# Attention over channels and an expert layer in Strassen form: extras of step 0 moved, sums of batch two made early, the last pair in eight plain products

## Reference

```python
def _attn_ref(q, k, v, tau):                    # q, k, v: 2 x 6016 x 256
    qn = q / (np.linalg.norm(q, axis=1, keepdims=True) + 1e-06)
    kn = k / (np.linalg.norm(k, axis=1, keepdims=True) + 1e-06)
    s = kn.transpose(0, 2, 1) @ qn / tau        # 256 x 256 for each batch
    s = s - s.max(-1, keepdims=True)
    a = np.exp(s)
    a /= a.sum(-1, keepdims=True) + 1e-09
    return (v @ a).astype(np.float32)
def _moe_ref(x, w_in, w_out):                   # x: 12032 x 256, w_in: 256 x 2048
    h = x @ w_in
    g = h * (1.0 / (1.0 + np.exp(-h)))
    return (g @ w_out).astype(np.float32)
```

## Time and profile before

| | |
|---|---|
| Time, median of 3 runs | 1074.22 us (1074.03 to 1078.78) |
| The profiled execution, its time | 1070.89 us |
| Its span | 1069.1 us |
| TensorE busy | 1034.2 us (97%) |
| VectorE busy | 934.1 us (87%) |
| ScalarE busy | 898.7 us (84%) |
| GpSimd busy | 297.6 us (28%) |
| DMA | 197.06 MB, mean 184 GB/s |

### The profile page before, as it was taken

One profiled execution on the slowest core, in us unless ns is written; L12 is line 12 of the kernel. 1 busy time (PEld: TensorE's weight loads), 2 busy tenths in 40 slices (PEclk: granted clock), 3 DMA queues, 4 the chain that ended last, 5 costly groups with the idle time before them and its releaser, 6 DMA issues.

```text
span 1069.1 us, 15160 instructions
## 1 busy us (share of the span) xinstructions
PE 1034.2 (97%) x4584; PEld 851.6 (80%) x4584; DVE 934.1 (87%) x1307; ACT 898.7 (84%) x1580; POOL 297.6 (28%) x323
## 2 busy tenths in 40 slices
PE   9999998989999999999978999999999999999997
PEld 8987776767888888888867777888888888888886
DVE  6887685689889899899899999899899899899898
ACT  7997676778898998898867788898898898988875
POOL 3695231143120121221273662121121211210100
PEclk9999999999999999999999999999999999999999
DMA  9993421397786885876975885885876876975742
GB/s 358 397 366 89 151 92 66 133 265 176 199 194 152 215 196 135 216 176 148 255 150 143 225 193 124 219 188 132 235 173 152 217 173 147 229 168 130 176 134 88
DMA packets 107921, 197.06 MB, mean 184 GB/s; under 512 B 9424, under 2 KB 42448, under 8 KB 107712
## 3 DMA queue, kind: packets, MB, share of 16 engines
q1 hardware_dynamic: 82720, 150.07, 43.2%
q0 software_dynamic: 24544, 45.17, 25.9%
q10 hardware_dynamic: 576, 0.85, 0.2%
HBM read 145.82 MB, written 50.23 MB: 183 GB/s over the span
## 4 chain that ended last, share of the span: by engine, by line
PE 71%; DVE 6%; ACT 3%; issue 3%; DMA 2%; SPq 1%; DVEq 0%; POOL 0%; ACTq 0%; POOLq 0%
PE ps_h L823 12%; PE ps_h L825 12%; PE ps_h L824 12%; PE ps_o L883 6%; PE ps_o L884 6%; PE ps_o L885 6%; PE ps_h L883 5%; PE ps_h L885 5%; PE ps_h L884 5%; DVE t_raw L1584 1%; DVE g_lo L1572 1%; DMA ring<-s_dram 1%; PE ps_o L870 1%; PE ps_o L872 1%; PE ps_o L874 1%
## 5 line engine op out<-in xcount | busy, mean ns | idle before, releaser
L1572 DVE TENSOR_TENSOR g_lo<-h,g_hi 128x512 fp32r<-128x512 f32 (+1 forms) x296 | 205.4, 696 | 24.5 <-ACT g_hi L1206 23.2
L1206 ACT ACTIVATE g_hi<-h 128x512 fp32r<-128x512 f32 (+1 forms) x296 | 182.5, 620 | 10.2 <-PE ps_h L885 3.8
L648 POOL DMA_DIRECT2D out_t_dram<-fl_sb x70 | 61.6, 879 | 437.0 <-ACT fl_sb L1234 428.8
L823 PE MATMUL ps_h<-b_hi,a_hi_mid 128*128 128x512 f32 (+1 forms) x336 | 132.7, 395 | 6.1 <-ACT h L1183 3.1
L825 PE MATMUL ps_h<-b_hi,a_lo_mid 128*128 128x512 f32 (+1 forms) x336 | 130.9, 390 | 0.0
L824 PE MATMUL ps_h<-b_lo,a_hi_mid 128*128 128x512 f32 (+1 forms) x336 | 130.7, 389 | 0.0
L1558 DVE TENSOR_TENSOR h<-ps_h,w 128x512 f32<-128x512 f32 (+1 forms) x96 | 65.2, 679 | 61.5 <-PE ps_h L825 41.7
L883 PE MATMUL ps_h<-g_hi,ring 128*128 128x512 f32 (+1 forms) x264 | 103.7, 393 | 13.5 <-DVE g_lo L1572 7.2
L1606 DVE TENSOR_TENSOR gx_lo<-t_raw,gx_hi 128x1024 fp32r<-128x1024 f32 (+1 forms) x88 | 107.8, 1225 | 0.6 <-ACT gx_hi L1213 0.6
L1584 DVE TENSOR_TENSOR t_raw<-h 128x1024 f32<-128x1024 f32 (+1 forms) x88 | 107.4, 1221 | 0.0
L883 PE MATMUL ps_o<-gx_hi,ring 128*128 128x512 f32 (+1 forms) x264 | 102.2, 387 | 0.7 <-DVE gx_lo L1616 0.4
(11 more groups left out here) (217 smaller groups left out, 2772.7 us busy)
## 6 DMA issues: line engine op xcount, KB each, us to landing
ring<-s_dram SPq DMA_DIRECT2D x88, 640.0 KB, 5.0
ring<-s_dram SPq DMA_DIRECT2D x88, 256.0 KB, 3.1
out_t_dram<-fl_sb POOLq DMA_DIRECT2D x72, 256.0 KB, 6.2
x_raw<-v_t_dram SPq DMA_DIRECT2D x58, 256.0 KB, 4.4
x_raw<-v_t_dram POOLq DMA_DIRECT2D x45, 256.0 KB, 7.1
out_t_dram<-o_sb SPq DMA_DIRECT2D x27, 256.0 KB, 4.5
out_t_dram<-o_sb POOLq DMA_DIRECT2D x27, 256.0 KB, 6.0
qk<-q_dram SPq DMA_DIRECT2D x17, 384.0 KB, 11.0
```

Source lines behind the costliest of these rows:

```text
L823: nc.tensor.matmul(out, w_hi, x_hi, start=start, stop=False, skip_group_check=True)
L1206: nc.scalar.activation(g_hi[:, g, 0:tok], h[:, g, 0:tok], ACT.Copy).then_inc(hi[g], 1)
L1572: nc.vector.tensor_tensor(g_lo[:, g, 0:tok], h[:, g, 0:tok], g_hi[:, g, 0:tok].bitcast(F32), ALU.subtract).then_inc(lo[g], 1)
```

## The change

- probs_hi is there for each batch, and round_probs(1) stands three copies earlier.
- Step 0: split_a stands before make_c22 in every pair; the parts' splits stand ahead of make_c22 (PARTS_EARLY) or right behind it (PARTS_LATE), x's splits one or two pairs later. Part 6 is split at pair 9 (raw half behind split_h, sums behind split_t4) instead of pair 10, part 7 at pair 11 instead of 12.
- VectorE makes the sums of A of batch two for all pairs at once in pairs 1 and 2 (four operations); ScalarE's queue stores all seven blocks of each pair to a1_dram. In steps 5 and 6 SyncE loads the seven blocks straight into a_lo (ahead of the ring load), ScalarE rounds them (round_a1), VectorE splits them in place in one operation; GpSimd has no part in it.
- The outputs of step 0 have places of their own (fl, out_11, u_sum, out_10) instead of x_raw, and are stored behind load_x(2), one by one.
- x of the next step is loaded in pair 0 of a step instead of pair 7 of the one before; add_x_first stands in pair 1 instead of 0, add_x_second in pair 2 instead of 1; roundings and splits are spread anew, T4's split stands in pair 0.
- The last pair (95): eight plain products with A11, A21 (loaded into F3's place), and so on, without the sums t1 to t4; ScalarE's queue and SyncE store the four blocks in another order. The partial sums that the earlier pairs left in m1, m4 to m7 are combined on VectorE and GpSimd beside it.

```diff
+        A1_SPLIT_AT = (42, 44, 46, 48, 49, 50, 52, 54)
+        a1_split_at = {n: pair for pair, n in enumerate(A1_SPLIT_AT)}
+        a1_load_at = {max(n - 2, SWITCH + 1): pair for pair, n in enumerate(A1_SPLIT_AT)}
...
-        X_SECOND = (B11, B21, B22, T2, T1, T3, T4)
-        X_LATER = (B11, B21, T2, B22, T1, T3, T4)
+        X_LATER = (B11, T2, B21, T1, B22, T3, T4)
...
+                if n == LAST:
+                    sp.wait_ge(a21_stored, 16)
+                    sp.dma_start(ring[:, n % 2, :, 0:F3, :].bitcast(F32), s_dram[PAIRS - 1, :, :, 0:F3, :]).then_inc(
+                        ring_a[n % 2], 16)
+                    sp.dma_start(ring[:, n % 2, :, A21_RING, :].bitcast(F32), a21_dram).then_inc(ring_a[n % 2], 16)
+                    return
...
             def load_a1(pair):
-                sp.wait_ge(a_split, PAIRS)
-                if pair >= 2:
-                    sp.wait_ge(a1_split, pair - 1)
-                sp.dma_start(a1_raw[pair % 2][:], a1_dram[:, pair]).then_inc(a1_loaded[pair % 2], 16)
...
-            store_std_outputs()
-            sp.wait_ge(out_stored, 32)
+            sp.wait_ge(x_split, x_groups(1))
             load_x(2)
+            for t, c in ((1, 0), (1, 1), (0, 0), (0, 1)):
+                store_std_output(t, c)
             for n in range(FIRST + 2, PERIODS):
                 it, pair = divmod(n, PAIRS)
+                if n in a1_load_at:
+                    load_a1(a1_load_at[n])
                 load_ring_a(n)
-                if n == FIRST + 3:
+                if n == FIRST + 2:
                     store_part(6)
                     sp.wait_ge(part_stored, part_stored_by(6))
                     load_part(7)
-                if n == FIRST + 5:
+                if n == FIRST + 4:
                     store_part(7)
+                    sp.wait_ge(a21_made, 2)
+                    sp.dma_start(a21_dram, late_parts[:, 14:16, :]).then_inc(a21_stored, 16)
                 if it > 1 and pair == 0:
                     begin_c12(it - 1)
                 if it > 1 and pair == 1:
                     begin_c21(it - 1)
                 if it > 1 and pair == 5:
                     store_c22(it - 1)
-                load_ring_b(n)
-                if n + 1 in reload_at:
-                    load_a1(reload_at[n + 1])
-                if pair == PAIRS - 1 and it + 2 < ALL:
-                    sp.wait_ge(x_split, x_groups(it + 1))
-                    load_x(it + 2)
+                if pair == 0 and it + 1 < ALL:
+                    sp.wait_ge(x_split, x_groups(it))
+                    load_x(it + 1)
+                if n < LAST:
+                    load_ring_b(n)
...
+                if i == PAIRS - 1:
+                    nc.gpsimd.tensor_copy(a21_high.bitcast(F32R), a21).then_inc(a21_made, 1)
+                    pool.wait_ge(a21_made, 1)
+                    nc.gpsimd.tensor_tensor(a21_low.bitcast(F32R), a21, a21_high, ALU.subtract).then_inc(a21_made, 1)
...
+            add_x_first(2)
...
-                if pair == (0 if it > 1 else 2) and it + 1 < ALL:
+                if it > 1 and pair == 1 and it + 1 < ALL:
                     add_x_first(it + 1)
-                if pair == (1 if it > 1 else 3) and it + 1 < ALL:
+                if pair == 2 and it + 1 < ALL:
                     add_x_second(it + 1)
-                if pair == (5 if it > 1 else 6) and it + 1 < ALL:
+                if pair == 5 and it + 1 < ALL:
                     add_x_third(it + 1)
-                if n == FIRST + 4:
+                if n == FIRST + 2:
                     part(7)
-                if n in reload_at:
-                    prepare_a1(reload_at[n])
+            n = tokens_of(FINAL)[1]
+            pool.wait_ge(u_summed, FINAL)
+            pool.wait_ge(o7_copied, FINAL)
+            pool.wait_ge(c21_made, PERIODS)
+            nc.gpsimd.tensor_tensor(u[:, 0:n], u_sum[:, 0:n], o7[:, 0:n], ALU.add).then_inc(last_w, 1)
+            pool.wait_ge(last_nv, 1)
+            pool.wait_ge(c22_stored, 16 * (FINAL - 1))
+            nc.gpsimd.tensor_tensor(o4[:, 0:n], o3[:, 0:n], o7[:, 0:n], ALU.subtract).then_inc(last_w, 1)
...
+            def closing_products():
+                f_t1(LAST - 1)
+                f_t2(LAST - 1)
+                pe.wait_ge(ring_a[LAST % 2], 16 * ((LAST - FIRST) // 2 + 2))
+                pe.wait_ge(lo[H11], LAST + 1)
+                pe.wait_ge(o1_copied, FINAL)
+                last_pair(F1, H11, m1, False)
+                last_pair(A21_RING, H11, m4, False)
+                pe.wait_ge(lo[H22], LAST + 1)
+                last_pair(F2, H22, m3, False)
+                pe.wait_ge(lo[H12], FIRST + 1)
+                last_pair(F1, H12, m3, False).then_inc(last_summed, 1)
+                pe.wait_ge(lo[H21], LAST + 1)
+                last_pair(F2, H21, m1, False).then_inc(last_summed, 1)
+                last_pair(F4, H21, m4, False).then_inc(last_summed, 1)
+                pe.wait_ge(last_nv, 1)
+                last_pair(F4, H22, m5, True)
+                last_pair(A21_RING, H12, m5, False).then_inc(last_summed, 1)
...
+                if n == 1:
+                    act.wait_ge(a1_step, 2)
+                    act.dma_start(a1_dram[:, :, A12:A11 + 1], wp_raw[1][:, :, 0:3, :]).then_inc(a1_saved, 16)
+                    act.dma_start(a1_dram[:, :, S3], wp_raw[1][:, :, 3, :]).then_inc(a1_saved, 16)
+                if n == 2:
+                    act.wait_ge(a1_step, 4)
+                    act.dma_start(a1_dram[:, :, S1:S2 + 1], a1_sums[:, :, 0:2, :]).then_inc(a1_saved, 16)
+                    act.dma_start(a1_dram[:, :, S4], a1_sums[:, :, 2, :]).then_inc(a1_saved, 16)
...
+            def round_a1(pair):
+                act.wait_ge(a1_loaded[pair % 2], 16 * (pair // 2 + 1))
+                nc.scalar.activation(a_hi(pair), a_lo(pair).bitcast(F32), ACT.Copy).then_inc(a1_rounded, 1)
+
+            ROUND_X = {2: (B11,), 3: (T2, B21), 4: (T1,), 5: (B22,), 6: (T3,), 7: (T4,)}
...
+            SPLIT_X_FIRST = {5: (T1, T2), 6: (T3, T3), 7: (B11, B22)}
+            SPLIT_X_SECOND = {4: (B11, T2), 5: (B21,), 6: (T1,), 7: (B22, T3)}
+            SPLIT_X = {3: (B11,), 4: (T2,), 5: (B21,), 6: (T1,), 7: (B22, T3)}
...
+            def sum_a1_first():
+
+                dve.wait_ge(wp_copied, 2 * FOLDS)
+                a12, a22, a11, a21 = (wp_raw[1][:, :, i, :] for i in range(4))
+                nc.vector.tensor_tensor(a1_sums[:, :, 0, :], a22, a21, ALU.subtract).then_inc(a1_step, 1)
+                dve.wait_ge(a1_step, 1)
+                nc.vector.tensor_tensor(a21, a11, a21, ALU.subtract).then_inc(a1_step, 1)
+
+            def sum_a1_second():
+
+                a12, a22, a11, _ = (wp_raw[1][:, :, i, :] for i in range(4))
+                dve.wait_ge(a1_step, 2)
+                nc.vector.scalar_tensor_tensor(a1_sums[:, :, 1, :], a1_sums[:, :, 0, :], -1.0, a11, ALU.mult,
+                                               ALU.subtract).then_inc(a1_step, 1)
...
-            PARTS_AT = {1: 0, 2: 1, 3: 2, 4: 3, 6: 4, 8: 5, 10: 6, 12: 7}
+            PARTS_EARLY = {2: 1, 3: 2, 6: 4}
+            PARTS_LATE = {1: 0, 3: 3, 7: 5}
+            PARTS_AT = {FIRST + 1: 6, FIRST + 3: 7}
 
             def first_step(n):
                 if n:
@@ -1656,33 +1729,37 @@
                 if n == 0:
                     split_wo(0)
                     split_wo(1)
-                if 1 <= n < PAIRS - EARLY - 1:
+                if 1 <= n < PAIRS - 1:
                     split_a(0, n + 1)
+                if n in PARTS_EARLY:
+                    split_part(PARTS_EARLY[n])
+                if n == 1:
+                    sum_a1_first()
+                if n == 2:
+                    sum_a1_second()
+                if n in SPLIT_X_FIRST:
+                    split_x(1, *SPLIT_X_FIRST[n])
                 make_c22(n, TOK)
                 if n == 0:
                     split_wo(2)
                     split_wo(3)
+                if n in PARTS_LATE:
+                    split_part(PARTS_LATE[n])
                 split_h(n, TOK, H22)
                 make_c21(n, TOK)
                 split_h(n, TOK, H12)
-                if PAIRS - EARLY - 1 <= n < PAIRS - 1:
-                    split_a(0, n + 1)
                 if n < PAIRS - 2:
                     sum_a(0, n + 2)
-                if n in PARTS_AT:
-                    split_part(PARTS_AT[n])
-                if n in SPLIT_X_FIRST:
-                    split_x(1, *SPLIT_X_FIRST[n])
 
             def turning_pair(n):
                 split_h(n - 1, TOK, H11)
                 split_h(n - 1, TOK, H21)
+                split_x(1, T4, T4)
                 make_c22(n, TOK)
                 make_c21(n, TOK)
                 sum_t13(n, TOK)
                 split_h(n, TOK, H22)
                 split_h(n, TOK, H11)
-                split_part(PARTS_AT[n])
 
             def pair_step(n):
                 it, pair = divmod(n, PAIRS)
@@ -1691,6 +1768,8 @@
                     add_flush(n - 2)
                 sum_t2(n - 1, before)
```

(35 more changed lines are left out.)

## The result

| | before | after |
|---|---|---|
| Time, median of 4 runs | 1074.50 us (1074.03 to 1078.78) | 1107.21 us (1103.05 to 1111.35) |
| The profiled execution, its time | 1070.89 us | 1103.05 us |
| Its span | 1069.1 us | 1101.1 us |
| TensorE busy, mean granted clock | 1034.2 us, 0.995 | 1042.5 us, 0.981 |
| VectorE, GpSimd busy | 934.1, 297.6 us | 916.0, 246.8 us |

The ratio is 1.0295 (95%: 1.0249 to 1.0342): slower, by 32.7 us where 12.8 were forecast, and outside the forecast's range. The profiled executions differ by 32.2 us.

A forecast was written before the change was run, and what follows sets the result against it. TensorE, nearly always busy, was taken as the bound, so only longer stops of it count. Terms: 17.7 us won, 30.5 lost, 12.8 us slower; 1083.7 for the profiled execution, forecast 1087 us, range 1062 to 1102.

The forecast's parts named there:

- the x sums of steps 3 to 11: Steps 2 to 10: two more transfers ahead of the flushed tile's add delay flush; loss 30.5 us, between 7 and 48.
- The other bound of the forecast: Price of one GpSimd transfer ahead of the flush, from queue 0's bytes and time: 1.6 us; 1.2 was taken.
- Rival 2: x load in pair 0 delays c21's store and pair 1's ring, clock falls each step: 48 us, 1105; chance 0.12.
- The Trainium skill's fit: GpSimd transfer costs 2.0 us plus bytes over 436 GB/s: 0.6 us per transfer ahead, loss about 12 us.
- Pair 9: VectorE's early split waits for part 6, holding up ScalarE and TensorE: loss 8.3 us plus 1.7 for the clock, 10.0.
- Part 7: Two pairs after part 6, its split comes nearly in time: loss 1.5 us (0 to 3).
- Steps 5 and 6: A of batch two prepared without GpSimd, so VectorE is no longer slowed: gain 18 us (12 to 20).
- rival 3: Steps 5 and 6 are bound by VectorE itself and give back 8 instead of 18 us: 1097; chance 0.1.
- Step 0: Moved splits of A gain 6.1 us; sums of batch two and their stores lose 4.6 (1 to 7).
- The end: Last pair without sums t1 to t4 and their chain: gain 3.1 us (2 to 3.5).

The follow-up runs named there:

- two_ahead: The changed kernel with two of the three first x sums, not all three, ahead of the add of the flushed tile: 1082.4 us, one run.
- one_ahead: The changed kernel with one of the three first x sums, not all three, ahead of the add of the flushed tile: 1065.2 us, one run.
- before_sums_later: The kernel before with the first and second x sums of steps 3 to 11 issued one pair later, x loads unmoved: 1098.0 us, ratio 1.0216.
- store_first: one_ahead with SyncE's stores of part 5 and load of part 6 ahead of pair 9's two ring loads: 1055.3 us, one run.
- best: one_ahead with old part 6/7 splits, part 5 and three step 0 outputs stored before pair 9's ring loads, later second half of batch-two sums: 1048.7 us, 0.9749 of before.
- before_loads_later: before_sums_later with the x loads for steps 4 to 11 also moved from the eighth pair of the step before to the first pair: 1110.3 us, 1.0316 of before.

## Why the prediction fell short

- **Direction and places** were right: slower, flush stops in the fourth pair of nine steps, a stop at pair 9, gains in steps 0, 5, 6 and at the end. The forecast had the mechanism of each, and missed on sizes.
- **The step that failed is the x sums of steps 3 to 11**, as a size. It took 1.2 us for a transfer ahead of the add of fl, and 1.5 was measured: (36.4 - 9.5) / 9 / 2 between the two kernels, and the same between after, two_ahead and one_ahead. The other bound of the forecast, 1.6 us from queue 0's bytes and time, was the better one. The wait was 36.4 / 9 = 4.0 us and not 3.2, and with that stop the clock fell in eight places, not five. The nine pairs are 40.7 us over: 13.6 for the falls instead of 8.5, and 27.1 for the stops themselves instead of 22. Of this the kernel before had 7.9, but 6.6 of it in pairs 43 and 51, which the forecast counted among what steps 5 and 6 give back. So the term is 40.7 - 1.2 = 39.5 us, not 30.5.
- **3.3 us in before_sums_later** (29.6 / 9) looks like the forecast's 3.2, and is luck. There add_o7 went out 0.9 us earlier, which the forecast had not counted; with it the two transfers cost 29.6 / 9 - 9.5 / 9 + 0.9 = 3.1 us, again 1.5 each.
- **Rival 2** named 1105 us, 2 us from the median. The delay of c21's store by the loads is there, but it is no change from before, where the three sums of x made it. The forecast had said just that against the rival, and it held; the 48 us of the rival (falls in each step) came close through longer waits in GpSimd's queue. Whether the ring load of pair 1 is late through the loads was not tested.
- **The Trainium skill's fit** (DMA: Bandwidth & Descriptors, Anatomy of one DMA) would add 0.6 us for a transfer ahead; 1.5 was measured.
- **Pair 9**: 11.8 us more over, not 10.0; the stores took 7.4 us, where I used the 4.6 of the earlier trace rows. There the last ring load had gone out 2.2 us before the store (205.36 and 207.53), here 0.7 us (203.43 and 204.09); in store_first, with 0.6 us between them, it is 6.5 us. That the ring's bytes make the difference fits, but is not shown by itself. **Part 7** cost about 5.3 instead of 1.5 (pair 11 is at 4.6 us over though the 5.4 of before, the wait for x of step 2, are gone; pair 12 gave another 0.7). Together 5.6 us of the miss.
- **Steps 5 and 6** gave back 22.8 - 8.1 = 14.7 us, not 18, if the whole excess of before is set against that of after without pairs 43 and 51. Of these, 6.6 were in pairs 43 and 51, where the new order of the queue then made stops of its own, and only 8 lie in the other pairs. That is the size which rival 3 gave; its reason is another matter. The remainder of 8.1 us lies mostly in six of the eight pairs that split A (0.6 to 1.7 us over each), where rival 3 expected it, from VectorE's own load; that cause was not tested.
- **Step 0** gave 2.4 us instead of 1.5: the batch's sums, with ScalarE's stores, cost 2.8 us in pairs 1 and 2 together, not 4.6. Pair 2 has nearly all of it (2.9 us over, 0.3 before); in pair 1 it is 0.2 us.
- **The end** gave 2.3 us, not 3.1.
- Sum of the misses: 12.5 us in pairs 17 to 95, 6.3 in pairs 9 to 16, 0.8 at the end, -0.9 in step 0: 18.7 of the 19.4 us between 1083.7 and the profiled 1103.05.

What stays open: why pair 1 of step 0 is 3.4 to 3.6 us over in every version, and pair 4 1.3 to 2.0 in all but best; and which stops of TensorE make the clock fall (below).

## What to carry to other kernels

A queue issued by hand is a resource with an order: before moving transfers in it, list what stands behind them and who gets a buffer back from it. If two rows give two prices for a transfer, work the forecast out with both, above all where a longer stop also costs a fall of the clock. When transfers leave a place and others come to it, price the difference of the two, not the new ones alone. When an early start is planned for a buffer that circulates, follow the whole circle, the queue in which its store is issued included: that store here waited for a semaphore of another stream, not for bytes. And when a stop is removed, look for the one under it, which ended a little earlier and was not seen.

## What the runs showed of the hardware

A 256 KB accumulating transfer of GpSimd ahead of another in its queue delayed the landing of that one by about 1.5 us, 0.54 of it in issue (after, two_ahead, one_ahead, and before_sums_later when add_o7's earlier start is counted). A 256 KB store of SyncE landed after 2.1 us (median of ten) with neither three such transfers nor 1.5 MB of loads in the 10 us ahead of it, and after 2.7 to 2.9 with either.

TensorE's stops before p6 behind 300 us, in the kernel after, two_ahead, before_sums_later and before_loads_later together: of 19 stops of 2.5 us and more, 18 have 3.41 us or more at 1.2 GHz with or behind them; of six between 2.06 and 2.40 us, three have; of nine between 0.98 and 1.80 us, one has, after 1.75 us. So a stop costs its length, and in most cases 1.7 us more when it is 2.5 us or longer, but not surely.
